# A preamble rebuilt around its first 256 positions: gates, fold and first attention of a three-stage kernel

## What is computed

```
m_new = max(f + m, i);  f_stab = exp(f + m - m_new);  i_stab = exp(i - m_new)
C = f_stab * C + i_stab * (v k^T);   n = f_stab * n + i_stab * k
y_t = sigmoid(o_t) * (C q_t) / max(|n q_t|, 1)
```

## Time and profile before

| | |
|---|---|
| median of 3 runs | 852.54 us (852.46 to 853.27) |
| the profiled execution, its own time | 852.34 us |
| its span | 850.5 us |
| TensorE busy, matmul / weight load | 768.5 us / 744.7 us |
| VectorE busy | 626.3 us |
| ScalarE / GpSimd busy | 405.1 us / 313.8 us |
| mean granted TensorE clock | 0.975 |

### The profile page before, as it was taken

How to read it: one execution, slowest core, us unless ns; L and a number is a source line. 1 busy time by engine, 2 the same in 40 slices (tenths; PEclk the granted TensorE clock), 3 DMA queues, 4 the chain that set the end, 5 groups by cost and what they waited for, 6 DMA issues and landing times.

```text
span 850.5 us, 17185 instructions
## 1 busy us (share of the span) xinstructions
PE 768.5 (90%) x5762; PEld 744.7 (88%) x5762; DVE 626.3 (74%) x1010; ACT 405.1 (48%) x651; POOL 313.8 (37%) x296
## 2 busy tenths in 40 slices
PE   2798999999999999999999999805999999999994
PEld 1788999999999999999999999805999999999994
DVE  5575979888898989888888885436676777776750
ACT  3024454444444444444544445405566666766851
POOL 3352534534445453434444434323042333222111
PEclk9999999999999999999999999957899999999998
DMA  7942222223232322232222200057764335527200
GB/s 205 314 138 73 75 88 80 90 84 92 83 97 86 94 76 87 72 87 72 87 72 87 86 1 17 1 165 202 216 205 140 117 99 183 178 90 230 97 20 5
DMA packets 40273, 91.28 MB, mean 107 GB/s; under 512 B 6781, under 2 KB 24321, under 8 KB 38826
## 3 DMA queue, kind: packets, MB, share of 16 engines
q1 hardware_dynamic: 36346, 81.69, 31.2%
q0 software_dynamic: 3888, 9.08, 3.8%
HBM read 105.63 MB, written 9.33 MB: 135 GB/s over the span
## 4 chain that ended last, share of the span: by engine, by line
PE 74%; DVE 14%; DMA 4%; issue 3%; ACT 3%; SPq 1%; DVEq 0%; POOLq 0%; POOL 0%; ACTq 0%
PE bank L1251 17%; PE bank L1263 17%; PE bank L1439 12%; PE bank L1387 6%; PE bank L1206 5%; PE bank L1197 3%; PE bank L1401 3%; DVE w_l L1052 2%; PE bank L1214 2%; PE bank L1223 2%; DVE g_l L936 2%; ACT w_h L717 1%; DVE den L885 1%; DVE num L882 1%; DVE xs L896 1%
## 5 line engine op out<-in xcount | busy, mean ns | idle before, releaser
L509 POOL TENSOR_TENSOR g_t<-u_t,r_t 128x512 f32<-128x512 f32 x96 | 134.7, 1403 | 270.4 <-ACT u_t L644 270.4
L639 ACT ACTIVATE r_t<-bank,neg 128x512 f32<-128x512 f32 x96 | 66.0, 688 | 201.4 <-PE bank L1251 201.4
L1263 PE MATMUL bank<-wo_h,g_h 128*128 128x328 f32 x384 | 127.3, 332 | 1.2 <-DVE g_l L936 1.2
L1263 PE MATMUL bank<-wo_l,g_h 128*128 128x328 f32 x384 | 120.1, 313 | 0.0
L1263 PE MATMUL bank<-wo_h,g_l 128*128 128x328 f32 x384 | 120.1, 313 | 0.0
L930 DVE TENSOR_SCALAR u_t<-bank 128x512 f32<-128x512 f32 x96 | 65.4, 681 | 57.4 <-ACT r_t L639 36.9
L575 POOL DMA_INDIRECT out_x<-ob,idx_tok x31 | 37.4, 1206 | 181.6 <-ACT ob L753 170.0
L644 ACT ACTIVATE u_t<-u_t,half 128x512 f32<-128x512 f32 x96 | 69.5, 724 | 55.2 <-DVE u_t L930 55.2
L860 DVE TENSOR_TENSOR_SCAN W<-W,cst 128x512 f32<-128x512 f32 x48 | 84.2, 1757 | 1.9 <-DMA W<-decays 1.9
L1251 PE MATMUL bank<-xT_h,wi_h 128*128 (+1 forms) x384 | 77.8, 284 | 1.6 <-issue 1.6
L1439 PE MATMUL bank<-w_h,h_h 128*128 128x320 f32 x248 | 78.1, 315 | 1.1 <-DVE h_l L1072 1.1
(11 more groups left out here) (211 smaller groups left out, 1969.3 us busy)
## 6 DMA issues: line engine op xcount, KB each, us to landing
raw<-in_w SPq DMA_DIRECT2D x12, 1280.0 KB
W<-decays SPq DMA_DIRECT2D x24, 512.0 KB, 5.1
raw<-in_w SPq DMA_DIRECT2D x12, 1024.0 KB
raw2n<-in_w SPq DMA_DIRECT2D x7, 1280.0 KB
raw1n<-in_w SPq DMA_DIRECT2D x7, 1024.0 KB
raw<-in_w SPq DMA_DIRECT2D x24, 256.0 KB
qG<-in_q SPq DMA_DIRECT2D x24, 180.0 KB
qT<-in_qt SPq DMA_DIRECT2D x48, 80.0 KB
```

What stands on the lines that cost most here:

```text
L509: pool.tensor_tensor(g_t[p % 2][:, :], u_t[p % 2][:, :], r_t[p % 2][:, :], ALU.add).then_inc(sm["g_done"], 1)
L639: act.activation(r_t[p % 2][:, :], bank_h[p % 2][:, :], ACT.Relu, bias=neg1[:, 0:1]).then_inc(sm["r_done"], 1)
L1263: mm = pe.matmul(bank_acc[tt][:, 0:DL], l[p % 4][:, c], r[:, f, :], start=f == 0 and a == 0, stop=f == NT1 - 1 and a == 2)
```

## The change

- **Gates in two parts.** Positions 0 to 255 go first on DVE, ACT and TensorE (`gates(0)`), positions 256 to 767 later: `gates(1)` on DVE is the last step of `ahead`, its Exp, scan and transposes stand in stages 0 and 1 of block 0, and so do the store of the decays to DRAM and the read of W for unit 2.
- **The first two units' decays without DRAM.** DVE spreads 8 rows over a diagonal (`spread`), TensorE multiplies by ones into banks, and `scan_first` scans from the bank. Unit 0 has no `from_state`; its numerator is copied.
- **Separate banks** for the scores and results of unit 1, so that they don't wait for unit 0's.
- **Fold** moves: 4 steps in `ahead`, 6 in stage 0 and 6 in stage 1 of block 0.
- **Products of constants** (`keep_awake`): 128 x 512 bf16 matmuls whose result nobody reads, 18 at the start, 3 after the gates, 4 and 4 later.
- **w_in** is split in quarters of 512 columns: two in `ahead`, two in stages 1 and 2 of block 0. Its first half is loaded by ACT's queue at the very start.
- **The output gate** of units 0 and 1 is a Sigmoid on ACT in place of Exp, add, reciprocal.
- **DVE's w_out low halves**: the first in stage 0, the second in stage 5 of block 0 (before: in `ahead` and stage 3).

The core of the diff (FS_STEP, the count of gate steps that the store of the decays waits for, goes from 7 to 11). On SyncE and ScalarE:

```diff
             def first_loads(t):
                 load_unit(t, 0, False)
-                load_dense(0)
+                load_unit(t, 1, False)
+                load_turned(0)
+                load_dense_second(0)
+                load_turned(1)
+                load_dense(1)
+            def second_loads(t):
+                load_unit(t, 0, False)
                 sp.wait_ge(sm["gate_step"], FS_STEP)
...
                 load_decays(t, 0)
                 load_unit(t, 1)
+                sp.wait_ge(sm["gate_pe"], 6)
                 load_dense_second(1)
...
+            load_first_matrix(act, 0)
+                act.activation(to[:, :], oS[k][:, :], ACT.Sigmoid).then_inc(sm["e_ready"], 1)
```

On GpSimd:

```diff
             def ahead(t):
+                lo_dense(0)
+                pool.wait_ge(sm["gate_tr"], 3)
                 values(t, 0)
-                lo_dense(0, 0)
...
+                    if not prev and p in (1, 2):
+                        lo_dense(1 + p)
```

On VectorE:

```diff
+            def first_body(t):
+                    if p == 0:
+                        gates_end(1)
+                        gates_scan(1)
+                        lo_dense(0)
+                    elif p == 1:
+                        gates_out(1)
+                        scan(t + 1, 0, 0)
+                        weigh(t + 1, 0, 0)
+                        scan(t + 1, 0, 1)
+                        weigh(t + 1, 0, 1)
+                        lo_logits()
+                        sigmoid(t + 1, 0)
...
+                    else:
+                        sigmoid(t + 1, 1)
+                        lo_dense(1)
```

On TensorE:

```diff
+            pe.wait_ge(sm["prep"], 1)
+            keep_awake(18, bank_dc)
+            spread(0)
+            gates(0)
+            keep_awake(3, bank_num)
             def ahead(t):
+                scores(t, 0, (bank_s, bank_r))
+                spread(1)
+                intra(t, 0)
+                scores(t, 1, bank_h)
+                pe.wait_ge(sm["gate_tr"], 3)
                 to_state(t, 0)
+                keep_awake(4, bank_s)
+                pe.wait_ge(sm["scan_done"], 3)
+                intra(t, 1, bank_acc[0])
+                from_state(t, 1)
                 turn_x(t, 0)
+                to_state(t, 1)
+                fold(0, 4)
+                keep_awake(4, bank_h[0])
+                turn_x(t, 1)
...
-                    if not prev and p % 4 == 0:
-                        pe.wait_ge(sm["wi_lo"], p // 2 + 2)
+                    if not prev and p % 2 == 0:
+                        pe.wait_ge(sm["wi_lo"], p + 2)
                     if not prev and p % 4 == 2:
                         pe.wait_ge(sm["wo_lo"], p // 4 + 1)
                     if not prev and p == 2:
-                        pe.wait_ge(sm["wp_lo"], 1)
+                        pe.wait_ge(sm["wp_lo"], 2)
...
+                    if not prev and p == 1:
+                        gates(1)
+                    if not prev and p < 2:
+                        fold(4 + 6 * p, 10 + 6 * p)
```

More of the change, by code:

```diff
@@ L19 @@
 CH = S // P
-FS_STEP = 7
+CA = 2
+FS_STEP = 11
 NU = B * CH
@@ L688, in body @@
                     square_part(t, p)
+                    if not prev and p == 1:
+                        act.wait_ge(sm["x_ready"], 2)
                     if att and p in (1, 5):
@@ L981, in ahead @@
             def ahead(t):
-                sigmoid(t, 0)
-                scan(t, 0, 0)
-                scan(t, 0, 1)
-                weigh(t, 0, 0)
-                weigh(t, 0, 1)
-                scan(t, 1, 0)
-                scan(t, 1, 1)
+                for q in range(2):
+                    scan_first(0, q)
+                gates_out(0)
+                for q in range(2):
+                    weigh(t, 0, q, (bank_s, bank_r))
+                for q in range(2):
+                    scan_first(1, q)
@@ L989, in ahead @@
+                for q in range(2):
+                    weigh(t, 1, q, bank_h)
                 new_state(t, 0)
-                outputs(t, 0)
-                weigh(t, 1, 0)
+                outputs(t, 0, state=False)
+                outputs(t, 1, bank_acc[0], eS)
                 x_low(t, 0)
-                weigh(t, 1, 1)
-                sigmoid(t, 1)
-                lo_dense(0)
-                outputs(t, 1)
+                x_low(t, 1)
                 new_state(t, 1)
-                x_low(t, 1)
@@ L999, in ahead @@
-                lo_logits()
+                gates(1)
+            def first_body(t):
+                for p in range(NP1):
+                    if p == 4:
+                        x_low(t + 1, 0)
+                    clamp(t, p)
+                    if p == 7:
+                        x_low(t + 1, 1)
+                    if p == 5:
+                        weigh(t + 1, 1, 1)
+                    if p >= 1:
+                        g_low(t, p - 1)
+                    if p == 0:
[10 more added lines that the diff above has]
+                        sigmoid(t + 1, 0)
+                    elif p in (2, 6):
+                        outputs(t + 1, p // 4)
+                    elif p in (3, 7):
+                        new_state(t + 1, p // 4)
+                    elif p == 4:
+                        scan(t + 1, 1, 0)
+                        weigh(t + 1, 1, 0)
+                        scan(t + 1, 1, 1)
+                    else:
+                        sigmoid(t + 1, 1)
+                        lo_dense(1)
@@ L1001, in body @@
             def body(t, prev, att):
+                if not prev:
+                    first_body(t)
+                    return
                 for p in range(NP1):
@@ new lines, in spread, with keep_awake @@
+            def spread(k):
+                pe.wait_ge(sm["gx_ready"], k + 1)
+                for q in range(2):
+                    pe.matmul((bank_h, bank_acc)[k][q][:, :], ones_f[0:H, :], W[k][0:H, 4 * q:4 * q + 4, :].rearrange("p a b -> p (a b)"),
+                              start=True, stop=True).then_inc(sm["w_bc"], 1)
+            def keep_awake(n, to):
+                for _ in range(n):
+                    pe.matmul(to[:, :], ones_b[:, :], ones_b[:, :].unsqueeze(1).to_broadcast([P, 4, P]), start=True, stop=True)
@@ L1190, in scores @@
+            pe.wait_ge(sm["prep"], 1)
+            keep_awake(18, bank_dc)
+            pe.wait_ge(sm["const_in"], 16)
+            pe.wait_ge(sm["pool_set"], 1)
+            spread(0)
+            gates(0)
+            keep_awake(3, bank_num)
+            def scores(t, k, banks=(bank_s, bank_dc)):
                 u = t * 2 + k
```

308 lines of the change are left out of this document (176 added, 132 removed).

## The result

The changed kernel takes **862.54 us** (median of 9 runs, 857.87 to 866.38) against 853.27 of the kernel before in the same measurement: a ratio of 1.0083, with an interval of 1.0060 to 1.0107. It is slower. The forecast was 848.9 and the range ended at 857, so it missed in sign and in size. The profiled execution took 864.95 us (span 863.1). In its page TensorE's busy time rose from 768.5 to 790.8 us and its mean granted clock fell from 0.975 to 0.929, while DVE's busy time (626.0 against 626.3 us) and ACT's (407.1 against 405.1 us) stayed. More busy time at a lower clock, with hardly more work: TensorE is slower, somewhere.

What follows compares the result with a forecast made beforehand. A chain of waits was taken to bound the kernel ahead of 68.6 us, TensorE from block 0 on. 44.5 + 22.2 + 38.8 put block 1 at 105.5 against 109.06, so 848.9 us; own range 845 to 851, ends 839 and 857.

Steps and rivals of the forecast that it cites:

- The step that failed: T0 to first(0, 2): TensorE's own 18.4 us hidden under DVE's 22.2 if the clock rises.
- the fold inside block 0 pulls the clock down: Rival, block 0: slow fold lifts TensorE's sum to 26 or 30 us, passing DVE's 22.2; 855.2 us; chance 0.27.
- T0: First part: start of the first dense matmul, 68.6 us before, forecast at 44.5 with preamble matmuls at half rate.
- third part: From first(0, 2) to block 1: 31.1 us of work, 2.0 slow stage 2, 5.7 new stall, 38.8 in all.
- Gates and decays, DVE's way: T0 to first(0, 2): gates done at T0 + 8.2, W at T0 + 15.6, first(0, 2) at T0 + 22.2.
- POOL beside DVE's scans: Before first(0, 2): POOL's low part of w_in's third quarter slows DVE's scans by 2.2 us, bounds 0 and 3.5.
- Table load: ACT, Sigmoid to Exp in gates(1): 1.28 us; by the skill's 2.66 with drain, decays would be 1.4 later.
- slow stage 2: After first(0, 2): TensorE had stood idle, so stage 2 starts at half rate, 2.0 us, bounds 0 and 3.
- wait in stage 5: Ahead of first(0, 6): TensorE waits for DVE's moved second low half of w_out, a new stall of 5.7 us.
- wait for `xs` in stage 2: One of two old stalls, 0.45 and 1.65 us, forecast to vanish because sigmoid and outputs find TensorE later.
- The bank scans of units 0 and 1: By the skill's rule on two SBUF inputs, new scans that read a bank would not be disturbed by POOL.

Runs made afterwards that it cites:

- e1: Changed kernel, but ACT's queue issues w_in only once SP's array of constants has landed: 858.22 us, ratio 1.0063 to the kernel before.
- e2: Changed kernel with DVE's second w_out low half back in stage 3 and ACT's high half in stage 2: 855.33 us, ratio 1.0029 to the kernel before.
- e3: Changed kernel with eight products of constants ahead of each fold group in block 0: 865.08 us, ratio 1.0157 to the kernel before.
- e6: Changed kernel without the later 11 products of constants, keeping the first 18: 859.84 us, ratio 1.0099 to the kernel before.
- e11: e7 with POOL making w_in's last quarter ahead of stage 2's clamp, ACT's copy a stage earlier: 850.90 us, ratio 0.9969 to the kernel before.
- e5: Changed kernel with two of three matmuls left out of each of block 0's 12 fold steps: 862.22 us, ratio 1.0117 to the kernel before.
- e7: Changed kernel with the edits of e1, e2 and e6 together: 850.78 us, ratio 0.9984 to the kernel before.
- e9: Changed kernel with the edits of e1 and e2 together: 854.63 us, ratio 1.0017 to the kernel before.
- e10: e9 with four products of constants ahead of each block 0 fold group, three between steps: seven executions 850.6 to 853.6 us, four 868.6 to 872.3.
- e8: e9 with some 70 more products of constants between almost all thin pieces: four executions of 849.73, 852.47, 866.48 and 873.11 us.
- b1: Kernel before with only DVE's second w_out low half moved from stage 3 to stage 5 of block 0: 864.66 us, ratio 1.0122.

## Why the prediction was wrong, step by step

**The step that failed** is the sentence that TensorE's own 18.4 us between T0 and first(0, 2) are "hidden under that if the clock rises as it did from 68.6 to 74". It didn't rise. TensorE's own sum is, from the chain, first 3.75, scores 2.01, six fold steps 8.84, first 3.71, gates 1.58, six fold steps 8.84 and 1.01 of copying (ACT and DVE split the folded logits): 29.7, past DVE's 22.2. This is the rival "the fold inside block 0 pulls the clock down", with its bound of 30 "if all is slow". It had 0.27 and decided from T0 + 25.8. (The bound is 29.5 when added up, and that it met 29.7 is partly luck: it took 2.8 us for gates that took 1.58 at half rate, 1.6 for scores that took 2.01, and nothing for the copying. With its own T0 and third part the rival, too, gave only 855.2.) The row that should have weighed more was in the prediction: a fold of 11.7 us back to back at half rate. It was set against the rise in the first 5 us of block 0 of the kernel before, but there scores and then 16 more dense matmuls followed the first 16, and here scores and the fold. In the profiled execution of the changed kernel the clock was never raised between 11 and 82 us. The rival's words fit other executions better: in those of e1, e2, e3, e6 and e11 it rose 3 to 6 us after T0, behind the same first layer, and fell again under the fold; in those of e5, e7 and e9 it didn't rise there. What decides between the two isn't shown.

The steps in turn:

- **T0**: 44.5 predicted, 48.93 measured. From the first intra to T0 it took 24.6 us for the 25.6 of the sum, so half rate in `ahead` was right. The miss is the start of the first intra, 24.33 for 19. I named w_in as the last to come; it had landed by 10.8 (12 taken), and POOL was done with it at 16.4, while `Vp` started at 20.43, four microseconds idle. What came last was the constants array at 11.06, whose landing no term held, and behind it TensorE's own work at half rate: two spreads of 3.75 and 3.71 (the prediction had them done by 15.5 and gave them no time), gates 0.9, constants 1.4, scores 2.0. e1 showed the array's part at T0 to be 1.9 us, e6 the constants' 3.2.
- **Gates and decays, DVE's way**: right in size. T0 + 22.2 in e5, W at T0 + 15.5. That POOL's low part ended with it was not in the prediction.
- **POOL beside DVE's scans**: 2.2 taken (bounds 0 and 3.5). In the changed kernel the two scans took 2.07 and 3.34 us, the next pair, with POOL idle, 1.22 and 1.48: 2.7.
- **Table load**: 1.28 as in the earlier trace rows. The Exp started 0.02 us after it, and the instruction before had ended 0.02 us ahead of it. The Trainium skill, page "ScalarE: Activation LUTs", section "What ACT_TABLE_LOAD costs", has 2.66 us with a drain; here the switch cost 1.3, and the 1.4 us later decays didn't come. The changed kernel's ACT, from its timeline:

```profile
54.36 0.72 ACT L669 ACTIVATE u_t<-u_t,half 128x512 f32<-128x512 f32 x1 [0.82 <-DVE u_t L1011]
55.10 1.28 ACT L634 ACT_TABLE_LOAD   x1
56.40 1.06 ACT L634 ACTIVATE wo_r<-wo_r 32x1024 f32<-32x1024 f32 x1
```

- **From first(0, 2) to block 1**: 38.8 predicted, 43.1 measured. The slow stage 2 was 1.4 (2.0 taken). The wait in stage 5 was 6.29 (5.7 taken): the right mechanism, 0.6 undersized. Two things were missing: the clock falls in that wait, so that what follows, from first(0, 6) to block 1, costs 2.2 us more (13.0 against 10.8); and the wait for `xs` in stage 2, which I let vanish (1.65 in the earlier trace rows), was 2.16, since POOL's last quarter of w_in now met `den` there (`TENSOR_SCALAR den<-den` took 2.40 us). The first of them is what a reader can take from the earlier trace rows: there the clock had fallen within 5 us of TensorE's stop, and I forecast a stop of 5.7.
- **The bank scans of units 0 and 1** took 1.17 us each in the changed kernel, where POOL stood idle then. In e9 the second of the pair ran from 15.08 to 16.27, wholly inside POOL's subtraction, and the pair took the same 2.34 us, where in the changed kernel a scan of W beside such a subtraction took 3.34 for 1.48. The scans that read a bank are thus not disturbed, as the prediction drew from the rule:

```profile
13.94 2.34 DVE L931 TENSOR_TENSOR_SCAN W<-bank,cst 128x512 f32<-128x512 f32 x2 [1.18 <-PE bank L1315]
14.92 2.34 POOL L480 TENSOR_TENSOR wi_l<-wi_r,wi_h 128x1024 fp32r<-128x1024 f32 x1 [9.26 <-ACT wi_th L616]
```

That rule, of the Trainium skill's page "GPSIMD Engine Reference", section "1. Specifications", names instructions with two SBUF inputs and those in a 2-port perf mode. `TENSOR_SCALAR den<-den`, one tile in, was held as well: 1.19 us in e7 until POOL's next piece ended, 0.17 in e11. It isn't of the first kind; whether it is of the second no trace here tells.

The forecast's three terms would have been 48.9 + 22.2 + 38.8 = 109.9, no change, with T0 as measured. The failed step adds 7.5, the third term 4.3: 121.7.

## What to carry to other kernels

When thin matmuls whose rows show half rate are moved in among dense ones, price them, and the dense ones behind them, at half rate: that an engine is busy is no sign that its clock will rise. For a step that moves to a later stage, count from its consumer, add what the fall of the clock costs behind a wait of TensorE, and look which engine's long piece now lies beside a short instruction of another. A second queue doesn't add bandwidth: it takes it from the small transfer on which the chain hangs.

## What the runs showed that was not expected

- **The clock falls under a busy engine.** 0.91 and then 0.50 in e3 between 58 and 62 us, with 2.00 of 2.00 us busy, on matmuls of 8 columns. The Trainium skill's page "TensorE: Matmul & The Clock Gate", section "What's actually happening", ties the clock to how busy the engine has been; busy time as the profile counts it is not that measure, as e10's 76 us at 0.50 show too. In e2 it fell in the same way, from 0.97 to 0.50 at 58 us, with no constants near. What is counted in its place no run here settles.
- **One program, two levels.** e10 and e8 took from 850 to 873 us with mean clocks from 0.967 down to 0.927, and the profiled executions of e2, e7 and e9, which have the same or fewer constants than the changed kernel, show the fold of block 0 partly at full rate or not at all.
- **The constants array, 3.1 us before, took 9.3** with w_in issued from another engine's queue at the same time, and 96 KB of gates 6.2 in place of 2.2.
- **A wait of TensorE costs more than its length**: by the time block 1 starts, 6.24 us cost 12.3 in b1, and 6.29 cost 8.5 in the changed kernel.
